# Last unit's mask in pieces, and a new order of the steps around attention blocks 5 to 19

## The reference

```
scores = q k^T / 8, masked to a window of 32 keys back (heads 0-3)
         or to every fourth of 128 keys back (heads 4-7); softmax; times v
x   = attention output, 1152 tokens x 512
out = sum over e in 0..3 of p[:, e] * (relu(x @ w1[e]) @ w2[e])      # w1 512x1024
h   = out @ w_in                                                     # 512x2048
y   = ((a0 + a1 h + a2 h^2 + a3 h^3) / (1 + |b0||h| + |b1| h^2 + 1e-6)) @ w_out
```

## Time and profile before

| | us |
|---|---|
| median of 3 runs | 661.86 |
| the runs | 661.86, 662.43, 659.31 |
| the profiled execution | 664.65 |
| its span, first to last instruction | 662.6 |
| PE busy in it | 638.4 (96%) |
| VectorE, ScalarE, GpSimd busy | 396.3, 324.3, 290.7 |
| mean granted clock of PE | 0.987 |

### The profile page before, as it was taken

How to read it: one execution, slowest core, us unless ns; L and a number is a source line. 1 busy time by engine, 2 the same in 40 slices (tenths; PEclk the granted TensorE clock), 3 DMA queues, 4 the chain that set the end, 5 groups by cost and what they waited for, 6 DMA issues and landing times.

```text
span 662.6 us, 10696 instructions
## 1 busy us (share of the span) xinstructions
PE 638.4 (96%) x3984; PEld 564.1 (85%) x3984; DVE 396.3 (60%) x774; ACT 324.3 (49%) x752; POOL 290.7 (44%) x307
## 2 busy tenths in 40 slices
PE   8897878999999999999999999999999999999998
PEld 7685667898788889898898988989889999999996
DVE  6442564634665544623536433546988888889896
ACT  6773653334232234311244211235778787877774
POOL 6654454667311178320289200135632566642221
PEclk9997998999999999999999999999999999999999
DMA  9932210211100012110022100011260000001011
GB/s 279 307 109 98 70 66 33 96 63 65 65 33 0 1 65 96 63 34 1 33 64 95 64 2 1 32 36 62 95 223 1 1 0 2 1 0 48 1 48 47
DMA packets 22771, 39.76 MB, mean 60 GB/s; under 512 B 3584, under 2 KB 4224, under 8 KB 22720
## 3 DMA queue, kind: packets, MB, share of 16 engines
q1 hardware_dynamic: 22720, 39.09, 18.1%
HBM read 36.72 MB, written 2.36 MB: 59 GB/s over the span
## 4 chain that ended last, share of the span: by engine, by line
PE 84%; DVE 6%; ACT 3%; issue 3%; POOL 2%; DMA 1%; SPq 1%; POOLq 0%; ACTq 0%; DVEq 0%
PE banks L813 42%; PE banks L785 22%; PE banks L726 17%; ACT scratch L943 2%; DMA raw<-in_weights 1%; POOL scratch L1539 1%; PE banks L679 1%; DVE acc L1272 1%; PE banks L698 1%; POOL scratch L1508 1%; PE banks L849 1%; DVE stage L1354 1%; PE banks L669 0%; DVE s_stage L1289 0%; POOL w_lo L1565 0%
## 5 line engine op out<-in xcount | busy, mean ns | idle before, releaser
L813 PE MATMUL banks<-w_hi,h 128*128 128x512 f32 x512 | 169.8, 395 | 0.0
L1354 DVE TENSOR_TENSOR stage<-banks,stage 128x320 f32<-128x320 f32 (+1 forms) x140 | 64.0, 461 | 101.6 <-PE banks L785 97.4
L813 PEld LDWEIGHTS banks<-w_hi,h 128*128 128x128 f32 x512 | 96.1, 188 | 20.6
L813 PE MATMUL banks<-w_lo,h 128*128 128x512 f32 x256 | 101.2, 395 | 0.0
L1599 POOL TENSOR_TENSOR w_lo<-raw,w_hi 128x512 fp32r<-128x512 f32 x32 | 41.4, 1316 | 126.4 <-ACT w_hi L999 126.4
L1613 POOL TENSOR_TENSOR h_lo<-rational,h_hi 128x384 fp32r<-128x384 f32 x47 | 47.6, 1013 | 108.4 <-ACT h_hi L1163 108.4
L726 PE MATMUL banks<-x_hi,w_hi 128*128 128x384 f32 (+1 forms) x256 | 85.7, 335 | 0.2 <-DVE x_lo L1239 0.2
L1042 ACT ACTIVATE h<-stage 128x320 fp32r<-128x320 f32 (+1 forms) x84 | 37.0, 447 | 99.1 <-DVE stage L1354 98.8
L726 PE MATMUL banks<-x_lo,w_hi 128*128 128x384 f32 (+1 forms) x256 | 83.3, 325 | 0.0
L726 PE MATMUL banks<-x_hi,w_lo 128*128 128x384 f32 (+1 forms) x256 | 83.0, 324 | 0.0
L1565 POOL TENSOR_TENSOR w_lo<-raw,w_hi 128x512 fp32r<-128x512 f32 x40 | 52.8, 1332 | 43.9 <-ACT w_hi L979 43.2
(11 more groups left out here) (143 smaller groups left out, 1504.4 us busy)
## 6 DMA issues: line engine op xcount, KB each, us to landing
raw<-in_weights SPq DMA_DIRECT2D x48, 256.0 KB, 2.9
raw<-in_weights SPq DMA_DIRECT2D x20, 512.0 KB, 3.6
raw_last<-in_weights SPq DMA_DIRECT2D x16, 256.0 KB, 5.5
scratch<-in_v SPq DMA_DIRECT2D x16, 192.0 KB, 5.8
scratch<-in_qk_dil SPq DMA_DIRECT2D x8, 320.0 KB, 6.0
out_t<-acc SPq DMA_DIRECT2D x9, 256.0 KB, 2.1
scratch<-in_qk_plain SPq DMA_DIRECT2D x8, 272.0 KB, 5.4
scratch<-in_qk_rest SPq DMA_DIRECT2D x2, 256.0 KB, 3.3
```

The source lines that it names most:

```text
L813: last = nc.tensor.matmul(sum_bank(k, t), h[:, cols], w[:, f, :], start=f == 0 and i == 0, stop=f == FC - 1 and i == 2)
L1354: nc.vector.tensor_tensor(out, bank, to, ALU.add).then_inc(combined, 1)
```

## The change

GpSimd makes the rest mask in eight pieces (`rest_mask_band(a)` and `rest_mask_batches(a)` for a = 0 to 3, two selects each) at five places of its list. ScalarE's and VectorE's lists from block 5 to block 19 are written out in a new order, in which exponentials stand up to two blocks ahead, and transform steps and their casts at other places. One PE slot does its outer product before the turn. The steps of group g = 1 are spread over three places in each of three pairs. A weight load moves ahead of one load of v, and |b1| is taken later.

```
-W1_HIGH_AT = ((4,), (), (5,), (6,), (7,), (), (), ())
+OUTER_AHEAD = (1, 2)
+W1_HIGH_AT = ((), (), (4,), (5,), (6,), (7,), (), ())
-T_STEPS = {2: ((0, 0),), 3: ((0, 1),), 4: ((0, 2),), 5: ((0, 3),), FC - 1: ((1, 0), (1, 1), (1, 2))}
-T_STEPS_MIDDLE = {2: ((0, 3),), 3: ((1, 2),)}
-T_STEPS_END = {0: ((0, 0),), 1: ((0, 1), (0, 2)), 2: ((1, 0), (1, 1)), 3: ((1, 3),)}
+T_STEPS = (((), (), ()), ((0, 0), (0, 1), (0, 2)), ((0, 3), (1, 0), (1, 1)), ((1, 2), (1, 3), ()))
 # SP
+            load_raw1(0, 1)
             load_v(18)
-            load_raw1(0, 1)
 # PE, in the loop over a slot's blocks
+                        if (k, f) == OUTER_AHEAD:
+                            outer_of_slot(k, f)
+                            turn(w)
+                            scores(w + 2)
+                            values(w)
+                            continue
 # ACT, new list (in place of the loop over slots)
+            high_weights(0)      # W2 chunk 0
+            exponentials(6)
+            take_turned(5)
+            high(0, 2)
+            high(0, 3)
+            attention_hi(5)
+            high_weights(2)
...
+            high(1, 0)
+            steps_of_block(11)   # take_turned(11), exponentials(12), attention_hi(11)
+            exponentials(13)
+            high(1, 1)
+            take_turned(12)
+            attention_hi(12)
+            take_turned(13)
+            exponentials(14)
+            attention_hi(13)
+            exponentials(15)
+            high(1, 2)
+            take_turned(14)
+            high_pair(0, 0)
+            attention_hi(14)
...
+            high(1, 7)
+            high_pair(0, 2)
+            for t in ("T1", "T3", "T2"):
+                high_t(0, 1, t)
 ...                              # in the loop of pairs
                     snapshot(k, p)
+                    if k == KW and p == 0:
+                        high_t(0, 1, "T4")
                     high_quarter(k, p, "C11")
+                    high_t_of_step(t_step(k, p, 0))
 # DVE, new list
+            mask(6)
             invert(5)
-            mask(6)
+            maximum(6)
             attention_lo(4)
-            maximum(6)
+            invert(6)
             low(0, 2)
             low(0, 3)
-            invert(6)
...
+            mask(14)
+            maximum(14)
+            mask(15)
+            maximum(15)
+            invert(14)
+            attention_lo(13)
+            take_sums(0)
+            invert(15)
+            low(1, 2)
...
+            low(1, 3)
+            transform(0, 0, 0)
+            invert(16)
...
+            attention_lo(18)
+            transform(0, 0, 3)
+            attention_lo(19)
+            transform(0, 1, 0)
+            low(1, 7)
+            for step in (1, 2, 3):
+                transform(0, 1, step)
 # POOL
+            rest_mask_band(0); rest_mask_batches(0)
             normalise(5)
-            low_w1(0, 4)
...
+            rest_mask_band(1)
+            normalise(8)
...
+            rest_mask_batches(1)
+            normalise(9)
...
+            rest_mask_band(2)
+            normalise(10)
             low_w2(0, 5)
-            normalise(10)
-            make_rest_mask()
+            rest_mask_batches(2); rest_mask_band(3); rest_mask_batches(3)
+            end_rest_mask()
+            normalise(11)
             low_w2(0, 6)
-            normalise(11)
```

More of the change, by code:

```diff
@@ L185, in visits, with t_step @@
     return VISITS.get((k, f), ())
+def t_step(k, p, i):
+    return (T_STEPS[p][i] or None) if k == START[1] else None
 def expert_of(k):
@@ L1010, in high_t, with high_t_of_step @@
                 nc.scalar.activation(t_parts(g, d, t)[0], source, ACT.Copy).then_inc(t_hi_done, 1)
-            def high_t_of_step(g, d, step):
-                for t in T_OF_STEP[step]:
-                    high_t(g, d, t)
+            def high_t_of_step(chunk_and_step):
+                if chunk_and_step:
+                    d, step = chunk_and_step
+                    for t in T_OF_STEP[step]:
+                        high_t(1, d, t)
             def snapshot(k, p):
@@ L1067, in steps_of_block, with high_weights @@
                 attention_hi(w)
+            def high_weights(f):
+                for c in W1_HIGH_AT[f]:
+                    high_w1(c)
+                for c in W2_HIGH_AT[f]:
+                    high_w2(0, c)
             high(0, 0)
@@ L1073, in _ @@
             attention_hi(4)
[L1074 to L1095, removed]
@@ L1096, in _ @@
-            act.wait_ge(ab_in, 32)
-            nc.scalar.activation(b1_abs[:, :], b_sb[:, 1:2], ACT.Abs).then_inc(b1_ready, 1)
+            high_weights(0)
[5 more added lines that the diff above has]
+            high_weights(2)
+            for f in range(LAG, FC):
+                if f > LAG:
+                    high(0, f)
+                for w in visits(0, f):
+                    steps_of_block(w)
+                high_weights(f)
@@ new lines, in _ @@
+            high(1, 0)
[12 more added lines that the diff above has]
+            attention_hi(14)
+            high(1, 3)
+            steps_of_block(15)
+            high_t(0, 0, "T1")
+            high(1, 4)
@@ new lines, in _ @@
+            steps_of_block(16)
+            high_t(0, 0, "T3")
+            high_t(0, 0, "T2")
+            high_pair(0, 1)
+            high(1, 5)
+            steps_of_block(17)
+            high_t(0, 0, "T4")
+            exponentials(19)
+            high(1, 6)
+            take_turned(18)
+            attention_hi(18)
+            take_turned(19)
+            attention_hi(19)
+            high(1, 7)
+            high_pair(0, 2)
+            for t in ("T1", "T3", "T2"):
+                high_t(0, 1, t)
@@ L1112, in _ @@
                         high_x2(x2[0])
-                    if k == START[1]:
-                        for d, step in T_STEPS_MIDDLE.get(p, ()):
-                            high_t_of_step(1, d, step)
+                    high_t_of_step(t_step(k, p, 1))
                     high_quarter(k, p, "C21")
@@ L1123, in _ @@
                             high_w2(e + 1, c)
-                    if k == START[1]:
-                        for d, step in T_STEPS_END.get(p, ()):
-                            high_t_of_step(1, d, step)
+                    high_t_of_step(t_step(k, p, 2))
                     if x2[1:]:
@@ L1169, in keep_sums @@
                     nc.scalar.activation(acc[:, ITER[k][1] // P + t, :], ps_o[:, t, :], ACT.Copy).then_inc(kept, 1)
+            act.wait_ge(ab_in, 32)
+            nc.scalar.activation(b1_abs[:, :], b_sb[:, 1:2], ACT.Abs).then_inc(b1_ready, 1)
             high_pair(MOE, FP - 1)
@@ L1334, in transform, with transform_step @@
                     low_t(g, d, "T4", st1)
+            def transform_step(chunk_and_step):
+                if chunk_and_step:
+                    transform(1, *chunk_and_step)
             def combine(k, p, name):
@@ L1395, in _ @@
             low(0, 1)
+            mask(6)
             invert(5)
-            mask(6)
+            maximum(6)
             attention_lo(4)
-            maximum(6)
+            invert(6)
             low(0, 2)
             low(0, 3)
-            invert(6)
[L1403 to L1419, removed]
-                        low(k, f)
[L1421 to L1427, removed]
@@ L1428, in _ @@
-            transform(0, 1, 3)
+            for f in range(LAG, FC + 1):
+                k, f = divmod(f, FC)
+                for w in visits(k, f):
+                    mask(w + 1)
+                    attention_lo(w - 1)
+                    maximum(w + 1)
+                    if (k, f) != (0, LAG):
+                        low(k, f)
+                    invert(w + 1)
+            normalise_probs()
+            mask(13)
+            maximum(13)
+            attention_lo(11)
+            invert(13)
@@ new lines, in _ @@
+            low(1, 1)
+            attention_lo(12)
+            mask(14)
[7 more added lines that the diff above has]
+            low(1, 2)
+            mask(16)
+            maximum(16)
+            attention_lo(14)
+            low(1, 3)
+            transform(0, 0, 0)
+            invert(16)
+            mask(17)
+            attention_lo(15)
+            maximum(17)
@@ new lines, in _ @@
+            low(1, 4)
+            transform(0, 0, 1)
+            invert(17)
+            mask(18)
+            attention_lo(16)
+            maximum(18)
+            low(1, 5)
+            transform(0, 0, 2)
+            invert(18)
+            mask(19)
+            maximum(19)
+            attention_lo(17)
+            invert(19)
+            low(1, 6)
+            attention_lo(18)
[3 more added lines that the diff above has]
+            low(1, 7)
@@ L1434, in _ @@
                     combine(k, p, "U2")
+                    transform_step(t_step(k, p, 0))
                     low_quarter(k, p, "C11")
@@ L1440, in _ @@
                         low_x2(x2[0])
-                    if k == START[1]:
-                        for d, step in T_STEPS_MIDDLE.get(p, ()):
```

(55 more changed lines are left out.)

1 line of the change is left out of this document (removed).

## The result

The changed kernel takes 642.71 us (median of 4 runs, 641.84 to 644.64) against 662.14 us before (4 runs): a ratio of 0.9717, 95% interval 0.9678 to 0.9756, or 19.4 us less by the medians. A later comparison on another chip gave 642.95 us and 0.972 (0.9698 to 0.9741). Forecast were 639.4 us, range 635 to 649. The profiled execution took 643.32 us with a span of 641.5 us (664.65 and 662.6 before).

A forecast was written before the change was run, and what follows sets the result against it. PE was taken as the bound, busy 638.4 of 662.6 us. Gaps of 16.7 us plus half clock of 7.2, less 1.4 for stalls and meetings, gave 22.5 off the 661.86 us median: 639.4 us, range 635 to 649.

The forecast's parts named there:

- The bound and the two kinds of loss: PE bounds the kernel; only gaps in its stream and stretches at half clock (1.2 instead of 2.4 GHz) can be won back.
- The mask: Last unit's mask in eight pieces, block 10's normalisation earlier: PE gaps of 4.0 and 1.0 us before blocks 11 and 10 go.
- The crowding of GpSimd: Part of the crowded-queues rival: extra idle time per pair of selects makes GpSimd late; whole rival 648.7 us, chance 0.20.
- Early part: Block 6's exponentials ahead of block 5's copy, inversions ahead of low parts: 2.1 us gap and 1.5 us half clock go.
- predicted 0.15 us stall: Block 5's copy now stands behind block 6's exponentials; bounds 0 and 1.44 us, taken as 0.15 us.
- Slots: New order of blocks 12 to 19 with transforms moved: PE waits of 3.1 us for copies and 2.3 us for normalisations go.
- 0.4 us behind exponentials(15): New stall in slot (1, 2): values(14) stands behind ScalarE's exponentials(15); bounds 0 and 1.44 us, taken as 0.4 us.
- Spread: Second expert's transform steps spread over the pairs: PE waits of 1.5 and 0.7 us behind 125 us go.
- The snapshot: ScalarE's snapshot of the first Strassen product, taken before the last T4: PE's 2.0 us wait goes, about 0.8 us to spare.
- term for meetings of GpSimd and VectorE: Allowance of 0.8 us, bounds 0 and 10, for VectorE and GpSimd instructions excluding each other.
- The slack that I set against it: VectorE has about 3 us of slack per pair behind U2 and C22; a step beside GpSimd's casts, 3.2 us, just fits.
- The sum: Gaps 16.7 us plus half clock 7.2 us, less 1.4 us for new stalls and meetings: 22.5 us gained.

The follow-up runs named there:

- run 7: The kernel before with only block 6's exponentials ahead of block 5's copy, inversions ahead of low parts, and W1 casts a slot later: 659.05 us, ratio 0.9949.
- run 11: The changed kernel itself, unchanged, measured again on another chip: 642.95 us, 0.972 of the kernel before.
- run 6: The changed kernel with GpSimd's low parts of the third pair held back until VectorE has T2's low part of chunk 1: 644.95 us, ratio 0.9739.
- Runs 5: The changed kernel with ScalarE's snapshot of the first Strassen product taken right after T1's cast, ahead of the casts of T3 and T2: 641.9 us, ratio 0.9691.
- 9: The changed kernel with the third pair's low parts held back and ScalarE's casts of the fourth pair moved behind C12's high part: 640.66 us, ratio 0.9679.
- run 2: The changed kernel with the mask's sixteen selects in one piece between the cast of W2's chunk 5 and block 11's normalisation: 646.95 us, ratio 0.9771.

## Why the prediction was right, and where it was off

**The bound and the two kinds of loss: right.** The parts, each tried alone or undone, gave 7.8 (mask), 3.4 (early part), 4.0 (spread) and 5.8 us (slots), 21.0 together against 18.5 to 19.4 for the whole. Each is known to 1.3 to 3 us, so they add up as far as these runs can tell.

**The mask: right.** Predicted 4.0 + 1.0 us of gap and about 4 of half clock, measured 7.8 alone. The crowding of GpSimd did not come: two selects take 0.6 to 0.7 us.

**Early part: right.** 3.6 us predicted, 3.4 measured; the predicted turn at 27.25 us is at 27.30 us in run 7 and at 27.31 in run 11, and the predicted 0.15 us stall is there (0.15 to 0.17). Block 11's turn, predicted for about 50 us, is at 50.11 in run 11 and at 51.41 in the first profile, where block 4 turned 1.3 us later.

**Slots: right.** Of the 0.4 us behind exponentials(15) 0.19 us came, and 0.34 us at block 18, which I had not listed. The waits that came back when the slots were undone are 4.2 us, where the sum has 5.4.

**Spread: right, but for the size.** No wait behind 105 us; alone it gave 4.0 us where the sum has 2.2, and the rest is not explained. Additions of 1.4 us beside GpSimd's casts fit into the slack, as worked out.

**The snapshot: wrong.** "The 2.0 us go, with about 0.8 us to spare" failed. What failed is the term for meetings of GpSimd and VectorE, 0.8 us taken from bounds of 0 and 10, in the one place where VectorE has no time to spare. In the changed kernel, up to what T2 is cast from, they made VectorE's steps 2.6 us longer than in run 6 (8.73 against 6.14 us), over three times the 0.8 us to spare, and PE waited 2.2 us. Runs 5, 6 and 9 show it from three sides. The second product, predicted for about 89 us, came at 92.60 us, and at 90.76 in run 11. The rule of the Trainium skill that I weighed there (SBUF — State Buffer, "Who interferes with whom") is borne out: 2.02 us for a subtraction of 0.49 us, ending just after GpSimd's of 2.10 us. The slack that I set against it was right for the second expert and wrong for the first pair.

**The sum.** In the profiled executions PE's waits behind 20 us fall from 18.1 us (rows 1 to 3) to 4.1 us, 14.0 us, where the sum had 16.7 less 0.55. The difference is the snapshot. Half clock: one less the mean granted clock, 0.987, times 662.6 is 8.6 us, and nothing after it; I had 7.2. The first 20 us took 1.3 us more, which is the chance of these two executions. 14.0 + 8.6 - 1.3 = 21.3, and the execution is 21.3 us faster (22.5 predicted): close by luck, because a half clock larger than mine hid part of the snapshot's loss. That the medians moved by 19.4 only is the second miss: I took the half clock of that one execution off the median, but the mean clock of the kernel before lay between 0.986 and 0.995 in 31 other executions, most at 0.989 to 0.992, which is 5 to 7 us of it. With the mean over those 31, 0.9905, and 0.999 over the nine executions of the changed kernel, the half clock gives 5.8 us in place of 7.2, and 14.0 + 5.8 = 19.8. "The gain belongs to work that every run does" holds for the gaps and not for the clock.

## What to carry to other kernels

A gap of the bounding engine had the same length in every profile here; the half clock behind it is a term of its own that differed between executions, so it should be taken from several runs' mean clocks and not from one trace. When GpSimd work is cut up and moved about, look at what VectorE does with two on-chip inputs in the same microseconds, and let the long GpSimd instruction wait where the one of VectorE is on the path. An engine with a strict list passes a delay on to whatever stands behind it: a held-back operation needs its consumer's place in the other list moved too.

## What the runs showed of the hardware

VectorE does not run slower beside GpSimd; it stands until GpSimd is done. The subtraction of 2.02 us began 0.43 us after GpSimd's and ended 0.35 us after it. Four more operations met GpSimd's between 90.7 and 94.6 us in the changed kernel, took 0.91 to 1.01 us instead of 0.49, and ended 0.34 to 0.36 us after it.

The clock fell behind some idle times of PE and not behind others of the same length. After 2.07 us in the kernel before it was 0.65 from 30 to 32 us. After the snapshot's wait it was 0.71 and 0.50 in run 2 (2.25 us), and 1.00 in the changed kernel (2.22 us). Behind the gap of 4.00 to 4.02 us the slot took 7.88, 5.89 and 6.61 us in three profiles, against 4.45 us with the gap filled. The changed kernel keeps one such wait, and its slowest execution, of 644.64 us, has a mean clock of 0.997, so some half clock was left in it; no trace shows where.

The first 20 us, the same instructions of PE in all these kernels, end (turn of block 4) between 19.10 and 21.74 us, which alone is 2.6 us of difference between executions.
